# The second layer's first tile also computes its four hidden blocks with narrower weights (126, 112, 96 columns) and with 256 tokens

## The chip, the core and the metric

The kernel runs on one core of a Trainium2 chip. The metric is the device time in microseconds (us), the median of three runs. On this core TensorE does the products and writes them to PSUM, VectorE (DVE), ScalarE (ACT) and GpSimd (POOL) do the elementwise work, and SyncE (SP) starts the transfers.

## The reference, cut to what matters

Three layers follow each other: a gated linear attention, a gated MLP, and a mixture of four experts in which every token goes through every expert. The change lies in the last of them:

```python
def _moe2_ref(x, domain_probs, w1, w2):          # x 3072 x 384, w1 4 x 384 x 1024, w2 4 x 1024 x 384
    p = domain_probs / (domain_probs.sum(-1, keepdims=True) + 1e-09)
    out = np.zeros((N, D), dtype=np.float32)
    for e in range(E):
        h = np.maximum(x @ w1[e], 0.0)
        out += p[:, e:e + 1] * (h @ w2[e])
    return out
```

## The kernel before, in words

The attention and the MLP (which the kernel's names call layer 1) run interleaved first, in eight tiles of 384 tokens; the mixture of experts (layer 2) follows. Each value that enters a large product is split into a high part, which the product's operand type fp32r keeps, and a low part, the remainder. So `x @ w` is three products: high by high, high by low and low by high (`SPLITS`, line 66).

Layer 2 makes eight passes, one for each half of the hidden width of each of four experts (`expert`, line 658). A pass goes over six tiles of 512 tokens. For each tile TensorE computes four hidden blocks (`first`, line 622: three slices of the model width by three splits, that is nine products with weights of 128 columns against 512 tokens), and between them four result blocks of the tile before (`second`, line 632: twelve products, 384 wide). Each block has its own PSUM bank: `hidden_banks` is (5, 6, 0, 1).

Behind each hidden block, ACT takes the relu as the high part (line 820) and DVE makes the low part (line 993). DVE adds the results to `acc` (line 985). The tokens of a tile are split by ACT (`split_x`, line 781) and by POOL (line 1094); those of the second tile by ACT and by DVE (line 1004).

The first tile of layer 2 is special, and the change lies there. Its blocks 0 and 1 are computed before the last output group of layer 1 (line 593, nine products), by the argument `ahead` of line 675; blocks 2 and 3 come after that group, at the start of `expert(0, alone=True)`. No result block stands between these four. Then TensorE waits for the last copy of layer 1 (`x2_ready`), which is ACT's line 760, and goes on with the second tile: its tokens must be split (`xsh_ready`, `xsl_ready`), and its block 0 waits in `first` (line 624) until DVE has made the first low part of the tile before (`rl_ready`).

Each engine runs its own instructions in order. A product in the trace is a pair: a weight load (LDWEIGHTS, engine "PEld") and the product itself (MATMUL, engine "PE").

Of the kernel before, what the change touches and what calls it, by code (L numbers as in the profile page):

```python
# [33 lines left out]
P = 128  # L34
B, H, S, D = 4, 8, 768, 48
DM = H * D
KD = DM // P
# [25 lines left out]
TILES2 = N // T2  # L63
PASSES = E * (F2 // FH)

SPLITS = ((0, 0), (0, 1), (1, 0))

# [139 lines left out]
def nth(e, c, j, per, extra):  # L209

    return e * (2 * TILES2 * per) + j * (2 * per) + (c * per + extra)


def wait_count(eng, sem, n):

    if not isinstance(n, int) or n > 0:
        eng.wait_ge(sem, n)
# [10 lines left out]
def attention_moe_program(nc, qk, alpha, v, rows, w_gate, w_val, w_out, probs, w1, w2, masks, eye, out):  # L228
    with ExitStack() as ctx:
# [4 lines left out]
        start = (nc.sbuf_base + 31) // 32 * 32  # L234
# [4 lines left out]
        def sb(name, shape, dt=F32):  # L239
            t = nc.alloc_sbuf_tensor_at(name, shape, dt, offset=top[0])  # L240
            top[0] += (int(np.prod(shape[1:])) * 4 + 31) // 32 * 32
            assert top[0] <= start + slab_bytes, (name, top[0] - start - slab_bytes)
            return t
# [37 lines left out]
        W1 = [[sb(f"W1_0{c}", [P, KD, FH], F32R) for c in "hl"]]  # L281
        W2 = [[sb(f"W2_0{c}", [P, FCH, DM], F32R) for c in "hl"]]
        XS = [[sb(f"XS_0{c}", [P, KD, T2], F32R) for c in "hl"]]
# [25 lines left out]
        PS = ctx.enter_context(nc.psum_tensor("PS", [P, 8, 512], F32))  # L309
        gate_bank, value_bank, out_bank0, att_bank0 = 0, 1, 2, 5  # L310
        hidden_banks = (5, 6, 0, 1)
# [200 lines left out]
        def _(pe):  # L512
# [57 lines left out]
            def group(i, tc, kind, f):  # L570
# [3 lines left out]
                if kind in ("gate", "value"):  # L574
# [6 lines left out]
                    for n in range(KD):  # L581
                        for w, x in SPLITS:
                            mm = pe.matmul(PS[:, bank, 0:T1], W[w][:, n, f * P:(f + 1) * P], xT[p][x][:, n, :],  # L583
                                           start=(n == 0 and (w, x) == SPLITS[0]), stop=(n == KD - 1 and (w, x) == SPLITS[-1]))
                    mm.then_inc(done, 1)
# [5 lines left out]
                for n in range(KD):  # L591
                    for w, x in SPLITS:
                        mm = pe.matmul(PS[:, out_bank0 + n, 0:T1], WO[w][:, f, n * P:(n + 1) * P], hs[f % 2][x][:],  # L593
                                       start=(f == 0 and (w, x) == SPLITS[0]), stop=(f == FC1 - 1 and (w, x) == SPLITS[-1]))
                mm.then_inc(out_done, 1)
# [26 lines left out]
            def first(e, c, j, f):  # L622

                wait_count(pe, rl_ready, nth(e, c, j, FCH, f + 1 - FCH))
                for n in range(KD):
                    for w, x in SPLITS:
                        mm = pe.matmul(PS[:, hidden_banks[f], :], W1[c // TILES2][w][:, n, f * P:(f + 1) * P],  # L627
                                       XS[c % 2][x][:, n, :],
                                       start=(n == 0 and (w, x) == SPLITS[0]), stop=(n == KD - 1 and (w, x) == SPLITS[-1]))
                mm.then_inc(first_done, 1)  # L630
# [11 lines left out]
            def tile2(e, c, j=0, alone=False, pieces=range(FCH)):  # L642

                if c % TILES2 == 0 and 0 in pieces:
                    pe.wait_ge(w1_ready, e * 2 + (c // TILES2 + 1))
                pe.wait_ge(xsh_ready, nth(e, c, j, 1, 1))
                pe.wait_ge(xsl_ready, nth(e, c, j, 1, 1))
                for f in pieces:
                    first(e, c, j, f)
                    if alone:  # L650
                        continue
                    if f == 0:
                        if (c - 1) % TILES2 == 0:
                            pe.wait_ge(w2_ready, e * 2 + ((c - 1) // TILES2 + 1))
                        pe.wait_ge(rl_ready, nth(e, c, j, FCH, 0))
                    second(e, c - 1, j, f)
# [561 lines left out]
```

## Time and profile before

| | us |
|---|---|
| Time, median of 3 runs (lowest to highest) | 1490.44 (1489.59 to 1491.31) |
| Time of the profiled execution | 1493.83 |
| Its span, from first to last instruction | 1492.0 |
| TensorE products busy in it | 1438.6 (96%) |
| Span from 686 us on (layer 2) | 806.0 |
| TensorE products busy in layer 2 | 803.04 |

A program on one core is timed here by its whole device time; the profile's span is the part between its first and last instruction. Records of products overlap: a product's record lasts 0.33 or 0.39 us while the next one starts 0.17 or 0.23 us after it. So the pace is read from starts, not from durations.

### The profile page before, as it was taken

The page shows a single profiled execution, that of the slowest core. Times are in us where ns is not written, and L with a number is a line of the kernel's source. Part 1 is how long each engine was busy: PE and PEld are TensorE (multiplying, and loading weights), DVE is VectorE, ACT ScalarE, POOL GpSimd, SP SyncE. Part 2 cuts the span into 40 slices and gives each one's busy share as a digit, 9 for nine tenths or more (in the row PEclk, how much of TensorE's full clock was granted, in tenths as well). Part 3 has the DMA queues.
Part 4 walks back from the last instruction along what each step waited for, and adds up shares of the span by engine and source line. Part 5 has one row for each costly group of instructions (what it writes and reads, how often), then busy time and mean ns, then how long its engine had stood idle before and what let it go on. Part 6 is the DMA issues. An engine that isn't in the chain of part 4 may idle for free.

```text
span 1492.0 us, 25792 instructions
## 1 busy us (share of the span) xinstructions
PE 1438.6 (96%) x10296; PEld 1327.3 (89%) x10296; DVE 620.4 (42%) x908; ACT 501.0 (34%) x975; POOL 597.8 (40%) x570
## 2 busy tenths in 40 slices
PE   3799999999999999999999999999999999999999
PEld 3688999898999898999999999999999999999998
DVE  8766654646455555312333333333333333333332
ACT  5554444545445445322222222222222222222220
POOL 7666454544444535254423413323234133242120
PEclk9999999999999999999999999999999999999999
DMA  6512122112121212100001001010010010100011
GB/s 229 188 51 102 51 84 70 68 67 70 66 88 52 93 60 83 43 22 22 0 1 43 0 1 43 0 43 1 1 42 0 0 42 0 42 0 0 19 44 63
DMA packets 31115, 70.70 MB, mean 47 GB/s; under 512 B 5168, under 2 KB 14128, under 8 KB 31024
## 3 DMA queue, kind: packets, MB, share of 16 engines
q1 hardware_dynamic: 31024, 69.43, 13.6%
q8 instruction: 64, 1.05, 0.3%
q14 instruction: 27, 0.22, 0.0%
HBM read 64.70 MB, written 4.72 MB: 47 GB/s over the span
## 4 chain that ended last, share of the span: by engine, by line
PE 89%; DVE 5%; issue 2%; POOL 2%; ACT 1%; DMA 1%; SPq 0%; DVEq 0%; ACTq 0%; POOLq 0%
PE PS L637 27%; PE PS L627 27%; PE PS L583 19%; PE PS L593 9%; PE PS L531 3%; PE PS L554 1%; DVE KQ L861 1%; PE PS L550 1%; ACT QX L738 1%; PE PS L534 1%; DVE near L866 1%; DMA V<-in_v 1%; DVE KQ L846 1%; DVE TOT L855 1%; DMA KQ<-in_qk 0%
## 5 line engine op out<-in xcount | busy, mean ns | idle before, releaser
L1094 POOL TENSOR_TENSOR XS_0l<-x2T,XS_0h 128x1536 fp32r<-128x1536 f32 x24 | 84.4, 3516 | 261.5 <-ACT XS_0h L781 261.5
L985 DVE SCALAR_TENSOR_TENSOR acc<-PS,prob,acc 128x384 f32<-128x384 f32 x192 | 118.7, 618 | 160.5 <-PE PS L637 160.5
L1094 POOL TENSOR_TENSOR XS_1l<-x2T,XS_1h 128x1536 fp32r<-128x1536 f32 x23 | 80.7, 3509 | 250.6 <-ACT XS_1h L781 250.6
L738 ACT ACTIVATE QX<-KQ 48x256 f32<-48x256 f32 x288 | 120.8, 419 | 139.5 <-DVE KQ L846 102.9
L820 ACT ACTIVATE H_1h<-PS 128x512 fp32r<-128x512 f32 x96 | 57.4, 598 | 309.9 <-PE PS L627 309.9
L820 ACT ACTIVATE H_0h<-PS 128x512 fp32r<-128x512 f32 x96 | 57.2, 598 | 297.3 <-PE PS L627 297.2
L846 DVE TENSOR_TENSOR KQ<-KQ,TOT 112x512 f32<-112x512 f32 (+1 forms) x144 | 126.9, 891 | 66.2 <-PE PS L531 37.7
L993 DVE SCALAR_TENSOR_TENSOR H_1l<-PS,H_1h 128x512 fp32r<-128x512 f32 x96 | 66.4, 691 | 195.8 <-ACT H_1h L820 195.8
L993 DVE SCALAR_TENSOR_TENSOR H_0l<-PS,H_0h 128x512 fp32r<-128x512 f32 x96 | 66.1, 691 | 187.4 <-ACT H_0h L820 187.4
L531 PE MATMUL PS<-QX,KQ 112*64 112x64 f32 x1920 | 86.7, 237 | 41.2 <-ACT QX L738 36.2
L531 PEld LDWEIGHTS PS<-QX,KQ 112*64 112x64 f32 x1920 | 73.2, 148 | 56.8 <-issue 27.9
L929 DVE TENSOR_TENSOR hid<-PS,hid 128x384 f32<-128x384 f32 x96 | 53.5, 557 | 155.9 <-PE PS L583 152.8
L1063 POOL TENSOR_TENSOR hs0l<-hid,hs0h 128x384 fp32r<-128x384 f32 x48 | 52.7, 1098 | 125.0 <-ACT hs0h L755 125.0
L1063 POOL TENSOR_TENSOR hs1l<-hid,hs1h 128x384 fp32r<-128x384 f32 x48 | 49.2, 1025 | 129.9 <-ACT hs1h L755 129.9
L751 ACT ACTIVATE hid<-PS 128x384 f32<-128x384 f32 x96 | 47.1, 491 | 80.2 <-PE PS L583 79.2
L1024 POOL TENSOR_TENSOR TOT<-TOT 112x128 f32<-112x128 f32 (+1 forms) x144 | 56.9, 395 | 26.4 <-DVE TOT L855 17.0
L894 DVE COPY_PREDICATED AT<-mask,PS 128x512 f32<-128x512 int32 x72 | 65.9, 915 | 0.5
L637 PE MATMUL PS<-W_1l,H_0h 128*128 128x384 f32 x192 | 64.8, 337 | 0.0
L637 PE MATMUL PS<-W_0l,H_1h 128*128 128x384 f32 x192 | 64.7, 337 | 0.0
L637 PE MATMUL PS<-W_1h,H_0h 128*128 128x384 f32 x192 | 64.7, 337 | 0.0
L637 PE MATMUL PS<-W_0h,H_1h 128*128 128x384 f32 x192 | 64.6, 337 | 0.0
L637 PE MATMUL PS<-W_0h,H_0h 128*128 128x384 f32 x192 | 64.6, 337 | 0.0
(152 smaller groups left out, 4137.1 us busy)
## 6 DMA issues: line engine op xcount, KB each, us to landing
row<-in_rows SPq DMA_DIRECT2D x24, 768.0 KB, 4.3
KQ<-in_qk SPq DMA_DIRECT2D x24, 448.0 KB, 4.1
V<-in_v SPq DMA_DIRECT2D x24, 384.0 KB, 4.8
rawA<-in_w SPq DMA_DIRECT2D x8, 768.0 KB, 4.8
rawB<-in_w SPq DMA_DIRECT2D x8, 768.0 KB, 6.4
A<-in_alpha SPq DMA_DIRECT2D x24, 224.0 KB, 2.7
out_y<-acc SPq DMA_DIRECT2D x5, 768.0 KB, 3.5
raw<-in_w_gate SPq DMA_DIRECT2D x3, 768.0 KB, 8.4
```

Source lines behind the costliest of these rows:

```text
L531: mm = pe.matmul(dst[mine, :, right], KQ[p][0:R, 1, a, mine], cols[:, :, right], start=True, stop=True)
L583: mm = pe.matmul(PS[:, bank, 0:T1], W[w][:, n, f * P:(f + 1) * P], xT[p][x][:, n, :], start=(n == 0 and (w, x) == SPLITS[0]), stop=(n == K ...
L593: mm = pe.matmul(PS[:, out_bank0 + n, 0:T1], WO[w][:, f, n * P:(n + 1) * P], hs[f % 2][x][:], start=(f == 0 and (w, x) == SPLITS[0]), stop ...
L627: mm = pe.matmul(PS[:, hidden_banks[f], :], W1[c // TILES2][w][:, n, f * P:(f + 1) * P], XS[c % 2][x][:, n, :], start=(n == 0 and (w, x) = ...
L637: mm = pe.matmul(PS[:, result_banks[u], 0:DM], H2[c % 2][x][:, f, u * P:(u + 1) * P], W2[c // TILES2 % 2][w][:, f, :], start=(f == 0 and ( ...
L738: done = nc.scalar.activation(QX[p][rows, :, g, :].rearrange("d a (n t) -> d a n t", t=2 << level), right, ACT.Copy)
L820: nc.scalar.activation(H2[c % 2][0][:, f, :], PS[:, hidden_banks[f], :], ACT.Relu).then_inc(rh_ready, 1)
L846: dve.tensor_tensor(x, x, y, ALU.mult).then_inc(kq_ready[p], 1)
L985: dve.scalar_tensor_tensor(out=acc[:, n, :], in0=PS[:, result_banks[u], 0:DM], scalar=weight, in1=acc[:, n, :], op0=ALU.mult, op1=ALU.add) ...
L993: dve.scalar_tensor_tensor(out=low, in0=PS[:, hidden_banks[f], :], scalar=0.0, in1=high.bitcast(F32), op0=ALU.max, op1=ALU.subtract).then_ ...
L1063: nc.gpsimd.tensor_tensor(hs[f % 2][1][:], hid[f % 2][:], hs[f % 2][0][:].bitcast(F32), ALU.subtract).then_inc(hl_ready, 1)
L1094: nc.gpsimd.tensor_tensor(XS[c % 2][1][:], x2T[:, :, at:at + T2], XS[c % 2][0][:].bitcast(F32), ALU.subtract).then_inc(xsl_ready, 1)
```

## The change

In `first`, after the wait on `rl_ready` and ahead of the usual nine products, the first tile of the first pass (expert 0, tile 0) also issues nine products for each of its four blocks: block 0 with the first 126 columns of its weight slices, block 1 with 112, block 2 with 96, all against 512 tokens, and block 3 with all 128 columns against the first 256 tokens. They write the same bank as the usual products; the usual group begins with `start=True`, and so overwrites what they left. No wait and no signal is added.

```diff
+FIRST_COLUMNS = ((126, 512), (112, 512), (96, 512), (128, 256))
 ...
             def first(e, c, j, f):
 
                 wait_count(pe, rl_ready, nth(e, c, j, FCH, f + 1 - FCH))
+                for cols, wide in FIRST_COLUMNS[f:f + 1] if isinstance(e, int) and e + c == 0 else ():
+                    for n in range(KD):
+                        for w, x in SPLITS:
+                            pe.matmul(PS[0:cols, hidden_banks[f], 0:wide], W1[c // TILES2][w][:, n, f * P:f * P + cols],
+                                      XS[c % 2][x][:, n, 0:wide], start=(n == 0 and (w, x) == SPLITS[0]),
+                                      stop=(n == KD - 1 and (w, x) == SPLITS[-1]))
                 for n in range(KD):
                     for w, x in SPLITS:
                         mm = pe.matmul(PS[:, hidden_banks[f], :], W1[c // TILES2][w][:, n, f * P:(f + 1) * P],
```

## Rows read from the trace of the kernel before

**Rows 1.** The page: TensorE's busy time, and its granted clock in 40 slices.
```profile
PE 1438.6 (96%) x10296; PEld 1327.3 (89%) x10296; DVE 620.4 (42%) x908; ACT 501.0 (34%) x975; POOL 597.8 (40%) x570
...
PEclk9999999999999999999999999999999999999999
```
**Rows 2.** The page: the chain that ended last, shares of the span by line.
```profile
PE PS L637 27%; PE PS L627 27%; PE PS L583 19%; PE PS L593 9%; PE PS L531 3%; PE PS L554 1%; DVE KQ L861 1%; PE PS L550 1%; ACT QX L738 1%; PE PS L534 1%; DVE near L866 1%; DMA V<-in_v 1%; DVE KQ L846 1%; DVE TOT L855 1%; DMA KQ<-in_qk 0%
```
**Rows 3.** Windows: layer 2 (busy us and count of each engine, clock, DMA).
```profile
686.00:1492.00 806.00, 803.04 (x4042) 728.27 (x4040) 252.79 (x385) 180.33 (x240) 250.11 (x151) 1.00 0.05 19
```
**Rows 4.** TensorE's waits after 686 us: total, times, longest.
```profile
PEld PS L627 <- issue: 0.4, 1, 0.4
```
**Rows 5.** Chain in order of time, 686 to 702 us: start, us, what.
```profile
686.05 4.09 PE PS L627 x18
690.14 1.56 PE PS L593 x9
691.70 4.09 PE PS L627 x18
695.79 0.05 issue
695.84 2.32 PE PS L627 x9
...
700.25 2.08 PE PS L627 x9
```
**Rows 6.** TensorE's timeline from 178.4 us: transposes in plain fp32 between products.
```profile
178.46 0.34 PE L593 MATMUL PS<-hs0h,WOl 128*128 128x384 f32 x1
178.64 0.49 PE L567 MATMUL PS<-ident,ynat 128*128 128x128 f32 x3
```
**Rows 7.** Groups by form: the transposes of line 567, busy us, mean ns.
```profile
L567 PE MATMUL PS<-ident,ynat 128*128 128x128 f32 x72 | 12.2, 278 | 2.0 <-DVE ynat L902 2.0
```
**Rows 8.** From 178.4 us too, weight loads.
```profile
178.46 0.43 PEld L567 LDWEIGHTS PS<-ident,ynat 128*128 128x128 f32 x3
```
**Rows 9.** The same kind of place with line 539, from 171.2 us.
```profile
171.24 0.34 PE L593 MATMUL PS<-hs1h,WOl 128*128 128x384 f32 x1
171.43 0.55 PE L539 MATMUL PS<-ident,KQ 112*128 112x112 f32 x4
```
**Rows 10.** From 300.7 us: a product, then one with 64 weight columns.
```profile
300.76 0.34 PE L593 MATMUL PS<-hs0h,WOl 128*128 128x384 f32 x1
301.03 0.30 PE L550 MATMUL PS<-ST,KQ 112*64 112x96 f32 x2
```
**Rows 11.** The weight loads there.
```profile
301.03 0.20 PEld L550 LDWEIGHTS PS<-ST,KQ 112*64 112x64 f32 x4 [0.25 <-DMA V<-in_v]
```
**Rows 12.** The weight load of the second tile's first product.
```profile
695.81 0.19 PEld L627 LDWEIGHTS PS<-XS_1h,W_0h 128*128 128x128 f32 x1 [0.44 <-issue]
```
**Rows 13.** TensorE's timeline around the second tile's first product: start, us.
```profile
695.40 0.39 PE L627 MATMUL PS<-XS_0h,W_0l 128*128 128x512 f32 x1
695.84 0.47 PE L627 MATMUL PS<-XS_1h,W_0h 128*128 128x512 f32 x1
696.15 0.40 PE L627 MATMUL PS<-XS_1l,W_0h 128*128 128x512 f32 x1
```
**Rows 14.** ACT's timeline, then DVE's, 690 to 697 us.
```profile
691.74 1.49 ACT L781 ACTIVATE XS_1h<-x2T 128x1536 fp32r<-128x1536 f32 x1 [5.97 <-PE PS L593]
693.13 1.12 ACT L760 ACTIVATE x2T<-PS 128x1152 f32<-128x1152 f32 x1
694.14 2.28 ACT L820 ACTIVATE H_0h<-PS 128x512 fp32r<-128x512 f32 x4
...
693.33 1.76 DVE L1004 TENSOR_TENSOR XS_1l<-x2T,XS_1h 128x1536 fp32r<-128x1536 f32 x1 [8.18 <-ACT XS_1h L781]
695.01 2.48 DVE L993 SCALAR_TENSOR_TENSOR H_0l<-PS,H_0h 128x512 fp32r<-128x512 f32 x4
```
**Rows 15.** The page: group of DVE's line 993: busy us, mean ns of one.
```profile
L993 DVE SCALAR_TENSOR_TENSOR H_0l<-PS,H_0h 128x512 fp32r<-128x512 f32 x96 | 66.1, 691 | 187.4 <-ACT H_0h L820 187.4
```

## The prediction

> **What bounds the kernel now.** I read the page first. TensorE's products are busy for 96% of the span at the full clock, and no other engine comes to half of it [rows 1]. The chain that ended last is made of TensorE's lines, with 27% each for the two lines of layer 2 [rows 2]. The windows then show layer 2 by itself: 803 of its 806 us are busy with products, at a granted clock of 1.00, which is the 2.4 GHz level [rows 3]. The list of waits has a single entry for TensorE in that whole stretch, 0.4 us at a weight load of line 627 [rows 4]. So from 686 us on TensorE is the bound with no slack under it: a product put in there moves the end by its own pace, and only that one wait can give something back. The chain in order of time shows the place of the change [rows 5]. Blocks 0 and 1 of the first tile take 4.09 us (18 products), then come layer 1's last nine products (1.56), blocks 2 and 3 (4.09), a short stop, and the second tile.
>
> **What is added.** The condition (a Python integer `e`, with e + c = 0) holds for the first tile of the first pass alone, once for each of four blocks: 4 x 9 = 36 products with their weight loads, 27 against 512 tokens and nine against 256. All are on TensorE, in a stretch where its starts follow each other without a gap. They sit on the path with their full price.
>
> Pace of the usual kinds: 4.09 / 18 = 0.2272 us for 512 tokens, 1.56 / 9 = 0.1733 for 384 [rows 5]. 128 tokens more cost 0.0539 us, so 384 of them are 0.1617, and 0.0116 is left that does not depend on the tokens: some 0.012 us for each pair of load and product.
>
> *Nine products against 256 tokens.* The columns are the usual 128. By the same line, 0.1733 - 0.0539 = 0.1194 us each, 1.07 us for nine. Could pairs follow each other that fast? The nearest row is a run of three transposes with 128 columns against 128: 0.49 us long [rows 6], one of them 0.278 [rows 7], so (0.49 - 0.28) / 2 = 0.105 us apart. That is just below 0.119, so I take 1.07. From below, the tokens alone are 9 x 0.108 = 0.97; from above, if a pair needed as long as one at 384 tokens, 9 x 0.1733 = 1.56.
>
> *27 products against 512 tokens with 126, 112 and 96 columns.* If the number of columns did not matter they would cost 27 x 0.2272 = 6.13 us: narrower weights leave columns of the array idle and do not shorten the stream of tokens. What may change is the load. No row of this kernel shows a load of fp32r weights with fewer than 128 columns, so I bound it from both sides.
> - From below: the load costs nothing, and the fixed 0.012 goes too: 27 x 0.2156 = 5.82 us.
> - The nearest row with another kind of load: the three plain fp32 transposes after a 384-token product. Their first load starts with that product, at 178.46 [rows 8], and the transpose starts 0.18 us after it [rows 6], where the usual distance is 0.173; with line 539 it is 0.19 [rows 9]. So a full-width load of the other type is hidden beside the running product but for some 0.01 us more than usual. 27 x 0.01 = 0.27.
> - From above: a load that cannot start until the stream before it has ended. The trace has one with 64 columns, where load and product start together in the records, 0.27 us after the product before [rows 10, 11], that is 0.10 us above the usual 0.173. The one exposed load of layer 2 agrees: from its start at 695.81 [rows 12] to the second product at 696.15 [rows 13] is 0.34 us, a product's 0.227 and 0.11 before it. 27 x 0.10 = 2.7 us.
>
> I take the middle one, because its load fills the whole array as these nearly do, whereas that of rows 10 changes over to half of it (and part of its wait is put down to a DMA). So the narrow products cost 6.13 + 0.27 = 6.40 us.
>
> Here the Trainium skill speaks against the change being that cheap. Its page "TensorE: Matmul & The Clock Gate", section "Weight-path perf modes — Fast Weight Load (FWL) and DoubleRow", says in my words that the fast load is used only when there are exactly 128 weight columns of a type other than fp32, and in theory loads them four times as fast. By that rule blocks 0 to 2 leave the fast load and block 3 keeps it, with the same page's "LDWEIGHTS" section giving columns / 1.2 in ns (105, 93 and 80 ns). Fully exposed, that would make the narrow products about 27 x 0.09 = 2.5 us dearer; fully hidden, nothing. No row here shows the fast load being left for this type.
>
> **What goes.** The one stop of layer 2. The first product of the second tile starts 0.44 us after the one before it and the next 0.31 after that [rows 13], against 0.227 each: 0.21 + 0.08 = 0.29 us lost (the chain has the same: 0.05 of issue, and 2.32 where a block otherwise takes 2.08 [rows 5]). The profile names no releaser; the code and the rows do. Block 0 of the second tile waits for the first low part of the first tile. After layer 1's last group ends (691.7), ACT splits the second tile until 693.2, DVE makes its low part from 693.33 to 695.09, and only then the first low part, from 695.01 on, 0.69 us long [rows 14, 15]: it is done at 695.70, and the load starts 0.11 later. This chain is 4.0 us long from the end of layer 1's last group, and TensorE has 4.09 us of products to lay beside it, of which the load ahead takes the margin. The added products of blocks 2 and 3 stand in the same place and make that 4.09 + 9 x 0.237 + 1.07 = 7.3 us. The wait goes: -0.29 us. The added products of blocks 0 and 1 come before layer 1's last group and shift both sides alike.
>
> What is late next? The low part of block 3, which the first result block waits for. ACT's 0.57 (2.28 / 4 [rows 14]) and DVE's 0.69 us [rows 15] after the end of block 3's last product, whose record of 0.39 us reaches 0.16 into the second tile, give 1.4 us; the load that wants it comes 8 products, 1.8 us, in. It holds, with 0.4 us to spare; without this cover it would cost a few tenths. ACT, DVE and POOL follow TensorE's signals afterwards as before and are idle most of the time. No transfer is touched: nothing of SP's and POOL's queues is moved past anything.
>
> **The sum.** 6.40 + 1.07 - 0.29 = +7.18 us. The profiled execution took 1493.83 us (span 1492.0 and 1.8 around it) and would take 1501.0. It lies 3.4 us above the median of the runs shown, and since nothing here scales with that difference, I carry the sum over: 1490.44 + 7.18 = 1497.6 us.
>
> **The rivals.**
> - *The load becomes a serial term, one step for each column.* The fixed 0.012 us may be a load that is never hidden and is fast for full-width weights only. If narrow weights went in one column at a time, at the pace at which tokens stream (0.0539 us for 128), 126, 112 and 96 columns would take 0.053, 0.047 and 0.040 us in place of the 0.012: 9 x (0.041 + 0.035 + 0.028) = 0.94 us above 6.13. Sum 6.13 + 0.94 + 1.07 - 0.29 = +7.85, time 1498.3. For it: the fixed part is there at both widths [rows 5]. Against it: in rows 8 a full-width load of another type, though nothing says that it is a fast one, was nearly hidden. By the fast-load rule of the page named above, four times 0.012 is 0.047 for a full-width load, which is what this rival takes for 112 columns; the rows neither bear out nor exclude it.
> - *Every narrow load is exposed as in rows 10.* 6.13 + 2.7 + 1.07 - 0.29 = +9.6, time 1500.1. For it: those are the only rows with fewer than 128 columns that follow an fp32r product. Against it: their switch to half the array, and a queue of TensorE that issues the next load at the start of the running product everywhere else.
> - *The narrow products leave the fast product too*, and stream at the pace of the plain fp32 rows: 0.105 us for 128 tokens [rows 6, 7], twice 0.054. Then 27 products cost 27 x 0.44 = 11.9, and with 1.07 and -0.29 the sum is +12.7, time 1503.1. Only the transposes speak for it, and these are bound by their loads as well as by their tokens.
> - *Not slower.* Layer 2 runs a little behind its own best pace: a hidden block takes 2.04 us in the quiet stretch (4.09 / 2) but 2.08 later [rows 5]. Over some 48 tiles with four such blocks these 0.04 us are 7.7 us. If the slow pace came from how the other engines' accesses fall against TensorE's, and the shift of 7 us moved them apart for good, it would give back up to 7.7 and end at 7.18 - 7.7 = -0.5, time 1489.9. It would have to give back over 4.2 us to leave "slower". Against it: the other engines wait for TensorE's signals, so they are shifted with it.
> - *The products are not there*, or write in parallel with others: they would need to be dropped or run beside the usual ones. They use the same array and bank, so I give this nothing of its own.
>
> **Chances.** My forecast 0.60 (1496.9 with the load free, to 1497.9), the serial load 0.19, the exposed load 0.10, the slow stream 0.07, not slower 0.04. Range: from 1496.4 (load free, and half a microsecond for the spread of the runs) to 1500.2, which takes in the exposed load. What a measurement of this kernel can tell from no change is about 0.2%, 3.0 us. Only the last rival comes under that: faster 0.01, same 0.03, slower 0.96.
>
> **What would show it right or wrong.** The rows of the new line should be 36 products and 36 loads between 685.9 and some 703 us. The distance of starts should be 0.23 to 0.24 us in the three narrow groups, about 2.13 us for nine, with no fall from 126 to 112 to 96, and 0.12 us in the fourth. Distances that fall with the columns (0.269, 0.262, 0.256) show the serial load, 0.32 or more the exposed one, 0.43 the slow stream. The wait of rows 4 should be gone and the distance at the second tile's start be 0.23. The rest of layer 2 should be as long as before. Any difference over 1 us outside the first 20 us of layer 2 would make the whole sum wrong.

## The result, and the profile after

The changed kernel takes 1498.54 us (median of three, 1498.43 to 1501.93) against 1490.44 (1489.59 to 1491.31): a ratio of 1.0062, 95% interval 1.0038 to 1.0085. The forecast was 1497.6 us, in a range of 1496.4 to 1500.2. A second comparison gave 1.0050 (1.0032 to 1.0067); it stands below with the experiments.

The medians differ by 8.1 us, and the two profiled executions by less: 1498.54 against 1493.83 us, spans 1496.8 against 1492.0. The trace says why. It has to be read in two parts, from the first product of the kernel to layer 2's first product, and from there to the last product of the kernel:

| us, from starts of products in the trace | before | after |
|---|---|---|
| first product to layer 2's first | 677.98 | 675.63 |
| layer 2's first product to the last of the kernel | 802.865 | 809.925 |

The trace of the kernel after has 36 products more (10332 against 10296). The second row is the change, +7.06 us. It is the same to the last digit in a second profile of the changed kernel (809.925). The first row is work that the change doesn't touch, and it scatters: over the thirteen profiles of this study it lies between 673.9 and 681.7 us.

The chain of the kernel after in order of time (start, us, what) answers to [rows 5]. Line 629 is the added product, 634 the usual hidden block (627 before), 594 layer 1's last output group (593 before), 644 the result block.

```profile
683.71 2.10 PE PS L629 x9
685.81 2.06 PE PS L634 x9
687.86 2.06 PE PS L629 x9
689.93 2.04 PE PS L634 x9
691.97 1.57 PE PS L594 x9
693.53 2.08 PE PS L629 x9
695.61 2.04 PE PS L634 x9
697.65 1.07 PE PS L629 x9
698.73 4.15 PE PS L634 x18
```

The four added groups stand there with 2.10 us (126 columns), 2.06 (112), 2.08 (96) and 1.07 (256 tokens), 7.31 in all. The piece of 4.15 us is block 3 of the first tile and block 0 of the second: there is no "issue" piece between them, and the list of waits has no entry for TensorE any more in layer 2 where [rows 4] had one. The starts around the second tile's first product (answering to [rows 13]) show the same:

```profile
700.40 0.39 PE L634 MATMUL PS<-XS_0h,W_0l 128*128 128x512 f32 x1
700.63 0.40 PE L634 MATMUL PS<-XS_1h,W_0h 128*128 128x512 f32 x1
700.87 0.40 PE L634 MATMUL PS<-XS_1l,W_0h 128*128 128x512 f32 x1
```

0.23 us from start to start in both places, where it was 0.44 and 0.31. ACT, then DVE, in the same stretch (answering to [rows 14]):

```profile
693.57 1.49 ACT L788 ACTIVATE XS_1h<-x2T 128x1536 fp32r<-128x1536 f32 x1 [10.14 <-PE PS L594]
694.97 1.11 ACT L767 ACTIVATE x2T<-PS 128x1152 f32<-128x1152 f32 x1
695.98 1.07 ACT L827 ACTIVATE H_0h<-PS 128x512 fp32r<-128x512 f32 x2
...
695.16 1.76 DVE L1011 TENSOR_TENSOR XS_1l<-x2T,XS_1h 128x1536 fp32r<-128x1536 f32 x1 [12.35 <-ACT XS_1h L788]
696.84 1.28 DVE L1000 SCALAR_TENSOR_TENSOR H_0l<-PS,H_0h 128x512 fp32r<-128x512 f32 x2
...
701.46 0.69 DVE L1000 SCALAR_TENSOR_TENSOR H_0l<-PS,H_0h 128x512 fp32r<-128x512 f32 x1 [2.45 <-ACT H_0h L827]
```

The split's low part is done at 696.9 and the first low part at 697.5, over 3 us ahead of the product at 700.63. The last low part ends at 702.15, and the weight load of the first result block, which needs it, starts at 702.48: what is late next stayed covered, with 0.3 us to spare. (The chain gives that block's start as 702.88, because it counts from the end of the record before; its first product starts at 702.71.)

The bill of layer 2, from starts in the two traces: added groups +7.31; the stop gone -0.28 (0.435 to 0.228 and 2.155 to 2.083 for the nine products behind it); the usual groups beside the added ones 8.21 instead of 8.18, +0.03. Sum, from the unrounded starts, +7.06.

### The profile page after: what moved, and what is told of

Read it like the earlier page. It is cut to its first block, busy times and chain, and to the rows that moved or that the text cites. A ratio compares the mean times of both kernels' runs of the same rounds, so it can differ in the third digit from the quotient of the medians.

```text
span 1496.8 us, 25864 instructions
## 1 busy us (share of the span) xinstructions
PE 1444.6 (97%) x10332; PEld 1332.2 (89%) x10332; DVE 622.8 (42%) x908; ACT 500.9 (33%) x975; POOL 597.0 (40%) x570
## 4 chain that ended last, share of the span: by engine, by line
PE 90%; DVE 5%; ACT 2%; issue 2%; DMA 0%; SPq 0%; DVEq 0%; ACTq 0%
PE PS L644 27%; PE PS L634 27%; PE PS L584 19%; PE PS L594 9%; PE PS L532 3%; PE PS L555 1%; ACT QX L745 1%; PE PS L551 1%; DVE KQ L868 1%; DVE near L873 1%; PE PS L535 1%; DVE KQ L853 1%; DVE TOT L862 1%; PE PS L540 1%; PE PS L629 0%
## 5 line engine op out<-in xcount | busy, mean ns | idle before, releaser
L853 DVE TENSOR_TENSOR KQ<-KQ,TOT 112x512 f32<-112x512 f32 (+1 forms) x144 | 130.2, 915 | 65.7 <-PE PS L532 37.6
```

What stands on the lines that cost most here:

```text
L853: dve.tensor_tensor(x, x, y, ALU.mult).then_inc(kq_ready[p], 1)
```

## The experiments

Eleven runs follow. "Layer 2" is from its first product to the last product of the kernel, from starts in the trace. Where a kernel ran only once, only the trace is used, since the first part of the kernel moves the device time by some us.

### Full width in all four blocks (one run)

```diff
-FIRST_COLUMNS = ((126, 512), (112, 512), (96, 512), (128, 256))
+FIRST_COLUMNS = ((128, 512), (128, 512), (128, 512), (128, 512))
```

> All four added blocks with 128 weight columns against 512 tokens, so that only the width differs from the changed kernel in blocks 0 to 2. Theory (the width of the weights does not matter while 512 tokens stream over them): the added groups of nine take 2.10, 2.06 and 2.08 us as they did with 126, 112 and 96 columns, each within 0.02, and the usual groups stay as they were. Rival (narrow loads pay a little that the neighbours hide, 1 to 4 ns a product): the full-width groups take 2.04 to 2.05 us, the best pace of this kernel, 0.03 to 0.05 less than the narrow ones. Block 3 takes 2.04 to 2.08 instead of 1.07. Layer 2 from its first product to its last: 809.9 + 1.0 = 810.9 us by the theory, 810.8 by the rival; the device time 1 us above the changed kernel's, within the spread of the first part of the kernel.

The chain of this kernel:

```profile
684.27 2.05 PE PS L629 x9
686.32 2.04 PE PS L634 x9
688.36 2.04 PE PS L629 x9
690.40 2.04 PE PS L634 x9
692.44 1.56 PE PS L594 x9
694.00 2.05 PE PS L629 x9
```

Layer 2 took 810.746 us. The rival was right by a small amount: full width takes 2.05, 2.04 and 2.05 us where 126, 112 and 96 columns took 2.10, 2.06 and 2.08. So the narrow groups took 6.23 - 6.15 = 0.09 us more together (unrounded), 0.003 for each of 27 products, and saved nothing. The sweep at the end puts in doubt that this is a price of the width.

### Narrow weights against 256 tokens (one run)

```diff
+FIRST_COLUMNS = (((126, 256), (128, 256)), ((112, 256),), ((96, 256), (64, 256)), ((128, 256),))
-                for cols, wide in FIRST_COLUMNS[f:f + 1] if ...
+                for cols, wide in FIRST_COLUMNS[f] if ...
```

> Added products against 256 tokens: block 0 with 126 and then 128 columns, block 1 with 112, block 2 with 96 and then 64, block 3 with 128. Theory (a load runs beside the product before it and only a fixed 0.012 us is left): 0.119 to 0.12 us from start to start for every width. Rival (a load of fewer than 128 columns is slower, and was hidden only because 512 tokens take 0.213 us): at 256 tokens, 0.107 us of streaming, the narrow widths come out longer than 0.12, up to 0.15 to 0.18 for 126, 112 and 96 columns, shrinking with the columns, while 128 columns stay at 0.12. A second rival for 64 columns (half of the array, as in the rows of line 550): the first product after a change of width class costs 0.10 us more.

The nine products of each kind took 1.058 us (126 columns), 1.080 (128), 1.057 (112), 1.045 (96), 1.030 (64) and 1.072 (128 again). From start to start that is 0.114 to 0.120 us. No narrow load is exposed at 256 tokens either; narrow is faster here by up to 0.006 us a product. Both rivals fell, and the theory's 0.119 to 0.12 us for every width missed by that much.

### Narrow weights against 128 tokens and less (one run)

```diff
+FIRST_COLUMNS = (((128, 128), (126, 128)), ((112, 128), (128, 192)), ((96, 128), (64, 128)), ((126, 192), (128, 64)))
```

The loop is changed as in the run before; this holds for every list of lists below.

> Added products against few tokens. Block 0: 128 columns x 128 tokens, 126 x 128. Block 1: 112 x 128, 128 x 192. Block 2: 96 x 128, 64 x 128. Block 3: 126 x 192, 128 x 64. Theory (fixed 0.012 us and the streaming alone, without a floor): 0.066 us from start to start at 128 tokens, 0.093 at 192, 0.039 at 64, whatever the columns. Rival A (a load and its product cannot follow the next pair faster than a floor of 0.105 to 0.11 us, as the transposes and the one exposed load of the kernel before): all of these at 0.105 to 0.11. Rival B (the floor exists and is higher for fewer than 128 columns): 128 columns 0.07 to 0.11, 126, 112 and 96 columns longer than 128 at the same tokens, in the order of their columns. Rival C (fp32r falls to a slower product under 256 tokens): 0.2 us or more for 128 and 192 tokens at every width.

This is the run that shows the load. The timeline of TensorE (start, record's length, what), all against 128 tokens, for 126, 112, 96 and 64 columns:

```profile
688.63 0.28 PE L629 MATMUL PS<-XS_0h,W_0h 128*126 128x128 f32 x1
...
689.18 0.27 PE L629 MATMUL PS<-XS_0h,W_0l 128*126 128x128 f32 x1
...
691.90 0.26 PE L629 MATMUL PS<-XS_0h,W_0l 128*112 128x128 f32 x1
...
692.40 0.26 PE L629 MATMUL PS<-XS_0l,W_0h 128*112 128x128 f32 x1
...
697.43 0.25 PE L629 MATMUL PS<-XS_0h,W_0l 128*96 128x128 f32 x1
...
697.85 0.25 PE L629 MATMUL PS<-XS_0l,W_0h 128*96 128x128 f32 x1
...
698.14 0.22 PE L629 MATMUL PS<-XS_0h,W_0l 128*64 128x128 f32 x1
...
698.50 0.22 PE L629 MATMUL PS<-XS_0h,W_0l 128*64 128x128 f32 x1
```

The pairs are five products apart (six for 64 columns): 0.55 / 5 = 0.110 us a product with 126 columns, 0.50 / 5 = 0.100 with 112, 0.42 / 5 = 0.084 with 96, 0.36 / 6 = 0.060 with 64. With 128 columns the median distance was 0.112 against 128 tokens, 0.111 against 192 and 0.112 against 64, so between these counts the tokens do not matter. The theory (0.066 us at 128 tokens, whatever the columns) fell. Rival A was right that a floor exists, and it was not one number: it goes with the columns, by about (0.112 - 0.084) / 32 = 0.0009 us each between 128 and 96.

That this floor is the load of the weights can be read from the start of the first group, with 128 columns against 128 tokens:

```profile
687.68 0.22 PE L629 MATMUL PS<-XS_0h,W_0h 128*128 128x128 f32 x1
687.68 0.19 PEld L629 LDWEIGHTS PS<-XS_0l,W_0h 128*128 128x128 f32 x1
687.74 0.28 PE L629 MATMUL PS<-XS_0l,W_0h 128*128 128x128 f32 x1
687.79 0.19 PEld L629 LDWEIGHTS PS<-XS_0h,W_0l 128*128 128x128 f32 x1
687.85 0.27 PE L629 MATMUL PS<-XS_0h,W_0l 128*128 128x128 f32 x1
```

The second product follows the first by only 0.058 us. The next load starts 0.11 us after the one before it, and from there on each product keeps that distance. So the products could go at 0.058, and the loads hold them back. With 64 columns the distance, 0.060, is about that of the tokens: each load there starts with the running product again, as against 512 tokens, so this row does not show how long a 64-column load takes. A load of 128 columns is no faster for its full width than one of 126 (0.112 and 0.110), so rival B had the order the wrong way round, and rival C fell.

Against 512 tokens, 0.216 us of streaming by the prediction's slope (4 x 0.0539), such a load has room beside the product before it. This is why the change's narrow weights neither save nor cost much. The rule weighed in the prediction (the Trainium skill, "TensorE: Matmul & The Clock Gate", "Weight-path perf modes — Fast Weight Load (FWL) and DoubleRow", which gives its four times as a theory for fp8) would make the 128-column load faster than that with 126 if it held for fp32r; the runs do not show it for this type, and the measurement decides. The same page's "LDWEIGHTS" section gives columns / 1.2 in ns: 106.7 for 128 and 80 for 96, and the trace agrees with its 112 and 84 to some 4 to 5 ns.

### The added products of blocks 0 and 1 alone (one run)

```diff
+FIRST_COLUMNS = (((126, 512),), ((112, 512),), (), ())
```

> The added products of blocks 0 and 1 alone (126 and 112 columns); none for blocks 2 and 3. Theory (the stop at the second tile's first product is a chain of 4.0 us that starts with the end of layer 1's last output group, and the added products of blocks 2 and 3 cover it): with none there, the stop is back, 0.44 us and 0.31 between the starts there, 0.29 us lost, and layer 2 takes 802.87 + 2.10 + 2.06 = 807.0 us from its first product to its last. Rival (the stop was a hiccup of issuing, or came from anything before layer 1's last group): no stop, 806.7 us.

```profile
694.86 1.56 PE PS L594 x9
696.42 4.09 PE PS L634 x18
700.51 0.04 issue
700.55 2.31 PE PS L634 x9
702.87 2.08 PE PS L644 x12
```

The stop is back, with 0.432 and 0.313 us between the starts, although TensorE had 4.16 us more to do ahead of layer 1's last group. So it belongs to what begins with that group's end, and the added products of blocks 2 and 3 are what covers it. Layer 2 took 806.41 us, 0.6 less than the 807.0 expected. That missing part lies behind the second tile's start: from there to the end it takes 792.29 us here, and 792.84 in the four other kernels above. See the last section.

### Four times the dose at 512 tokens (one run)

```diff
+FIRST_COLUMNS = (((126, 512),) * 4, ((128, 512),) * 4, ((96, 512),) * 4, ((64, 512), (64, 512), (32, 512), (32, 512)))
```

> Four times nine added products against 512 tokens in each block: block 0 with 126 columns, block 1 with 128, block 2 with 96, block 3 with 64 and 64 and 32 and 32. Theory (the load of any width is hidden under 512 tokens): every group of nine takes 2.04 to 2.10 us, so 36 with 126 columns take 8.2 to 8.4 and 36 with 96 columns the same; 16 groups add 33 to 33.5 us to layer 2, whose second-tile stop is gone: 802.9 + 33.2 - 0.3 = 835.8 us. Rival A (the fixed part is a quarter of a step per column, as the runs at 256 tokens hint: 128 columns 0.120, 64 columns 0.1135): 96 columns 0.2233 (2.01 us for nine), 64 columns 0.220 (1.98), 32 columns 0.2167 (1.95), 126 columns 2.04. Rival B (126 columns cost 0.233 us a product, 0.006 above full width, as in its one group so far, for as long as they go on): block 0 takes 36 x 0.233 = 8.39 us against 8.16 for block 1.

```profile
683.06 8.40 PE PS L629 x36
...
693.52 8.16 PE PS L629 x36
...
705.29 8.29 PE PS L629 x36
...
715.63 8.31 PE PS L629 x36
```

36 products took 8.40 us with 126 columns, 8.16 with 128, 8.29 with 96, 8.31 with 64 and 32. Layer 2 took 835.79 us, as expected (835.8). Rival B was right for 126 columns: 0.233 us each for as long as they go on. Rival A fell: fewer columns do not save time here.

### The dose at 256 tokens (one run)

```diff
+FIRST_COLUMNS = (((128, 256),) * 3 + ((64, 256),) * 3, ((32, 256),) * 3, ((96, 256),) * 3, ((112, 256),) * 3)
```

> Added products against 256 tokens, 27 in a row of each width: 128 and then 64 columns in block 0, 32 in block 1, 96 in block 2, 112 in block 3. Theory (a fixed part of 0.012 us whatever the columns): 0.119 us each, 3.22 us for 27 of any width. Rival (the fixed part goes with the columns, a quarter of a step for each): 128 columns 0.1200 (3.24 us for 27), 112 columns 0.1183 (3.20), 96 columns 0.1167 (3.15), 64 columns 0.1133 (3.06), 32 columns 0.110 (2.97). A third possibility (no order at all, 0.112 to 0.121 as in the mixed groups before): differences that don't follow the columns.

For nine products: 1.080 us with 128 columns, 1.060 with 112, 1.044 with 96, 1.020 with 64, as the rival has it to 0.01, but 1.060 with 32, where it wants 0.99. So the rival does not hold for all of them, and at 512 tokens it had the wrong sign. The theory's one time for all widths missed too. What sets these last 0.006 us a product stays open.

### The changed kernel again (seven runs)

> The changed kernel again, timed in five rounds against the kernel before on one chip. Theory (7.1 us come from layer 2, in every run, and anything else is the scatter of the first part of the kernel, whose half-clock windows and waits differ from run to run): +7.1 us between the medians give or take the scatter, a ratio of 1.0048 with an interval that may reach from 1.002 to 1.008; layer 2 809.9 us from its first product to its last in the profile. Rival (the change itself also makes the first part slower, by some 1 us, as 8.1 between the medians of three would have it): 1.0054 or more, and a first part longer than that of the kernel before.

1499.12 us (1497.32 to 1504.8, seven runs) against 1493.46 (1489.92 to 1496.94, eighteen runs); ratio 1.0050, 1.0032 to 1.0067. Layer 2 took 809.925 us in the profile, and the first part 678.03 us, as long as before's 677.98 in its own profile. The theory holds: 7.06 of 1490.44 us is 1.0047, inside both intervals, and the second comparison comes close to it. The rival's 1.0054 lies inside them too; what speaks against it is the first part, which isn't longer in the profile.

### Relu and low part of block 0 first, nothing added (twelve runs)

```diff
                 act.wait_ge(out_done, TILES1 * FC1)
+                act.wait_ge(first_done, 1)
+                nc.scalar.activation(H2[0][0][:, 0, :], PS[:, hidden_banks[0], :], ACT.Relu).then_inc(rh_ready, 1)
                 act.wait_ge(x2_ready, 2)
                 split_x(0, 1)
 ...
```

and the same for DVE's low part, ahead of its line 1004; both are left out of the usual loops.

> The kernel before with nothing added, but with the relu (ACT) and the low part (DVE) of the first tile's block 0 put ahead of the second tile's split. Theory (the stop of 0.29 us is the wait for the first low part at the end of a chain of 4.0 us): that low part is ready 1.4 us after layer 1's last group instead of 4.0, the split's low part takes its place at 0.6 + 1.5 + 1.8 = 3.9 us, and the stop shrinks to 0.1 us or none: layer 2 802.6 to 802.8 us from its first product to its last, the time the same as before (0.3 of 1490 us is 0.02%). Rival (the wait is one for the split, which now comes later by 0.6 us): the stop grows to 0.5 us or more, layer 2 803.2.

Ratio 1.0007 (0.9997 to 1.0017). Layer 2 took 802.858 us: the stop stayed (0.431 and 0.312 us), so the theory failed, and so did the rival's longer stop. DVE's timeline and the chain show what took over:

```profile
692.66 0.69 DVE L1005 SCALAR_TENSOR_TENSOR H_0l<-PS,H_0h 128x512 fp32r<-128x512 f32 x1 [7.22 <-ACT H_0h L810]
694.11 1.76 DVE L1009 TENSOR_TENSOR XS_1l<-x2T,XS_1h 128x1536 fp32r<-128x1536 f32 x1 [0.75 <-ACT XS_1h L781]
```
```profile
696.09 0.04 issue
696.13 2.31 PE PS L627 x9
```

The first low part was ready at 693.35, but the split's low part, which the relu in front of it had pushed back, now ended at 695.87. Both kernels can be compared by the time since the first product of block 2 (691.54 in the kernel before, 691.84 here). There the last low part needed ended 4.15 us after it, here the split's ended 4.04 after it, 0.12 us sooner; the load at which TensorE stops starts 4.27 us after it in both. Where the 0.12 us went stands in the trace's records of TensorE's own waiting instructions, of which no view is shown here: the wait for the split's low part comes one instruction ahead of that for the first low part. It goes through 0.04 us after the low part's end, the second waiting instruction follows 0.11 us later, and the load 0.08 after that. In the kernel before, the low part that came last was the second instruction's, which went through 0.04 us after it, with only the 0.08 behind. So moving one producer up pushed the other back to nearly the same time, and the order of the waits took the rest.

### The split in thirds as well (eleven runs)

```diff
-                split_x(0, 1)
+                for k in range(KD):
+                    nc.scalar.activation(XS[1][0][:, k, :], x2T[:, k, T2:2 * T2],
+                                         ACT.Copy).then_inc(xsh_ready if k == KD - 1 else xs_part, 1)
 ...
```

This stands on top of the edit of the run before, and DVE makes its low part in the same three pieces.

> The kernel before with nothing added, the relu and low part of the first tile's block 0 first (as in the run before this), and the second tile's split made in three pieces, one for each slice of the model width, so that DVE makes the low part of a slice while ACT makes the high part of the next. Theory (the stop ends with whichever comes last of the first low part and the split's low part; the one was moved before and the other, 4.04 us after layer 1's last group, took its place): the split's low part is now ready some 3.4 to 3.6 us after that group, before the 3.87 us at which TensorE could issue the load, and the stop is gone: 0.227 us from start to start there, layer 2 802.57 us from its first product to its last. Rival (the stop is TensorE's own cost of taking three waits in a row at that place): 0.43 and 0.31 us stay, 802.86. The time is the same as before in either case: 0.3 of 1490 us is 0.02%.

Ratio 1.0004 (0.9994 to 1.0014).

```profile
691.75 0.69 DVE L1008 SCALAR_TENSOR_TENSOR H_0l<-PS,H_0h 128x512 fp32r<-128x512 f32 x1 [7.22 <-ACT H_0h L811]
692.36 1.89 DVE L1013 TENSOR_TENSOR XS_1l<-x2T,XS_1h 128x512 fp32r<-128x512 f32 x3
695.25 1.89 DVE L998 SCALAR_TENSOR_TENSOR H_0l<-PS,H_0h 128x512 fp32r<-128x512 f32 x3 [1.00 <-ACT H_0h L825]
```
```profile
691.08 6.17 PE PS L628 x27
697.25 0.03 issue
697.28 2.32 PE PS L638 x12
```

The 27 products of blocks 2 and 3 and the second tile's block 0 now run without a stop: with both conditions ready, at 692.4 and 694.25, the wait is gone. That shows that it was these two, and the rival, a cost of TensorE's own, fell. But the stop has moved: the first result block waits for the fourth low part, which DVE ends at 697.14. The new stop loses as much as the old one (0.422 and 0.247 us, where 0.227 and 0.174 are usual: 0.27). Layer 2 took 802.232 us, 0.63 less than before, and 0.59 of that is the pace of the last section.

### Two relus first (eleven runs)

The run before, with block 1's relu and low part put ahead of the split too (two lines for each engine).

> As the run with the split in thirds, and the relu and low part of block 1 are also put ahead of the split, so that less is left for DVE behind it. Theory (in the run before, the first stop went and a second took its place: the first result block waits for the fourth low part, which DVE had ready 6.06 us after layer 1's last group, where TensorE could use it at 5.9): the fourth low part is now ready at 5.5 to 5.7 us and no stop is left, layer 2 802.23 - 0.27 = 801.96 us from its first product to its last. Rival (the last copy of layer 1 on ACT, pushed to 3.7 us, becomes what TensorE waits for at 3.87): a stop of 0.1 to 0.3 us at the second tile's first product, 802.1 to 802.3. The time stays within what can be told from the kernel before: 0.9 of 1490 us is 0.06%.

Ratio 0.9995 (0.9983 to 1.0007). The theory fell: a stop stands at the second tile's first product again, with 0.318 and 0.312 us between the starts, 0.18 lost, and layer 2 took 802.745 us. The size of the stop is the rival's, its cause is not. The view of waits puts it down to the last copy of layer 1:

```profile
PEld PS L628 <- ACT x2T L761: 0.3, 1, 0.3
```

But that entry goes by the load's own wait alone, and the split's low part (DVE) ended later than the copy (ACT):

```profile
697.29 1.13 ACT L761 ACTIVATE x2T<-PS 128x1152 f32<-128x1152 f32 x1
...
696.58 1.89 DVE L1016 TENSOR_TENSOR XS_1l<-x2T,XS_1h 128x512 fp32r<-128x512 f32 x3
```

The copy ends at 698.42, the split's low part at 698.47, and the load starts at 698.70, 0.23 us behind the low part, the same distance as in the run with one relu first (695.87 and 696.10). TensorE's waiting instruction for that low part goes through 0.04 us after its end, with the same 0.11 and 0.08 us behind it. The copy was only 0.05 us from being the last. The two relus and low parts put ahead had pushed both back. None of the three reordered kernels is faster than the one before by more than its measurement can tell.

### Token counts between 320 and 504 (one run)

```diff
+FIRST_COLUMNS = (((126, 504), (128, 504), (126, 448), (128, 448)), ((126, 384), (128, 384), (96, 384), (64, 384)),
+                 ((126, 320), (128, 320), (96, 320), (64, 320)), ((96, 448), (64, 448), (96, 504), (64, 504)))
```

> Added products with 126, 128, 96 and 64 columns against 504, 448, 384 and 320 tokens, nine of each. Theory (streaming plus a fixed 0.0133 us for 128 columns; at 512 tokens the narrower ones showed up to 0.0066 us more, at 256 up to 0.0066 us less): 128 columns 0.2233, 0.200, 0.1733 and 0.1467 us. For the others two readings: (A) the extra at 512 tokens belongs to the width, and is there at every token count above some point: 126 columns 0.230, 0.2065, 0.180, 0.153; (B) it comes from how load and stream fall against each other in steps of 0.0033 us, and changes with the token count without order: some of the counts show 126 columns at the pace of 128 or below it. In neither case is any load exposed: nothing above 0.24 us at 504 tokens.

Nine products took, in us, with 128 / 126 / 96 / 64 columns: 2.062 / 2.048 / 2.069 / 2.057 against 504 tokens, 1.824 / 1.815 / 1.830 / 1.825 against 448, 1.562 / 1.590 / 1.574 / 1.564 against 384, 1.313 / 1.318 / 1.318 / 1.315 against 320. Reading B fits: 126 columns are faster than 128 at 504 and 448 tokens and slower at 320, 384 and 512, so the 0.006 us at 512 are hardly the price of a narrow load. Each number is from a single group of nine, in one order, so an effect of the place in the row isn't excluded. All lie within 2% of full width. The theory's size missed at 504 tokens even for 128 columns: 2.01 us expected, 2.062 measured.

## Why the prediction was right, point by point

*The bound.* Right. Layer 2 paid for each added product in full, and beside the stop nothing else in it moved by more than 0.03 us.

*256 tokens, 1.07 us.* Measured 1.07. The doubt whether pairs can follow at 0.119 us was well placed: a 128-column load takes 0.111 to 0.112 us, as the run with few tokens shows, and that is the 0.11 of the exposed load of [rows 12, 13]. Whether the 0.105 of the transposes, which are of another type, is the same thing was not tried.

*27 narrow products, 6.40 us.* Measured 6.23. The mechanism was right (a load without a special width is hidden beside the product before it), and the term was mis-sized: I charged 0.01 us a product from the transposes, where 0.003 were measured against full width. The picture is simpler than the three cases that I bounded: a full-width load is no faster than a narrow one, and both are hidden from 256 tokens on, but for differences of some ns that stay open.

*The stop, -0.29 us.* Measured -0.28, and the cause named, the wait for the first low part, fits the kernel before: it ended at 695.70 and the split's low part 0.6 us ahead of it. The two runs that took the cover away or took the conditions away agree: without the added products of blocks 2 and 3 the stop is back, and with both conditions early it is gone. What I did not see is that the split stands in the same chain, so that moving the low part alone gains nothing. For the change itself this made no difference, since the added 3.15 us in blocks 2 and 3 cover both.

*What is late next.* Right: no wait came up. The low part of block 3 was ready 0.3 us before the load that needs it, where 0.4 were predicted.

*The sum, +7.18 us.* Measured +7.06 in layer 2. The difference of 8.1 us between the medians of three is this and 1 us of scatter in the first part; the range held it because of the room left for the exposed load, not because I had sized the scatter. That part is luck: in the second comparison the medians differ by 5.7 us, and 1490.44 + 5.7 would have been 1496.1, just under the range. I wrote off the 3.4 us between the profiled execution and the median, and should have read it as that scatter: the kernel before lay between 1489.3 and 1496.9 us over all its runs in this study.

*The rivals.* The serial load is out: it would show 0.269, 0.262 and 0.256 us, and 0.233, 0.229 and 0.231 were measured. The exposed load is out: 32 and 64 columns against 512 tokens took 0.230 to 0.232 us, where it asks for 0.32. So [rows 10] (64 columns of plain fp32) show something else; what it is wasn't tried. The slow stream is out. "Not slower" is out: 7.06 us stayed, though a change of pace like the one it spoke of exists in small (last section).

## What to carry to other kernels

A product added on the engine that is the bound costs its whole distance from start to start, here 0.23 us against 512 tokens. Making its weights narrower saves nothing at 512 tokens and costs next to nothing, as long as the stream is longer than the load, here 0.11 us for 128 columns. With 192 tokens and fewer a 128-column load set the pace, and at 128 tokens fewer columns did help, down to 64. When a stop is removed by moving one producer up, look for the other conditions that end within a few tenths of it, and for the order in which the waiting engine takes them: this stop was ended by the first low part, then by the split's, then (at another place) by the fourth low part, then by the split's again with layer 1's last copy 0.05 us behind it. Check the view of waits against the ends of all producers: it named the copy, which was not the last.

## What the runs showed of the hardware that was not expected

The distance between two equal products is not one number. For 512 tokens with 128 columns it lies between 224 and 236 ns in layer 2 of the kernel before, in patterns that depend on what stands around the products, and some patterns last as long as nothing disturbs them: 36 products at a mean of 233 ns with 126 columns, 230 with 96, and 227 with 128. Such a pattern can tip for a while. From the second result block to the end of the kernel the same instructions take 786.59 us in eleven of the thirteen profiles, to 0.001 us, and 786.00 in two: the kernel with added products in blocks 0 and 1 only, and the split in thirds. The whole difference arises in the first 80 us of that stretch, about the first pass; from there on the starts keep the same distance to 0.001 us. At its beginning the result blocks have 2.08 us instead of 2.09 in the chain, and the hidden blocks 2.06 instead of 2.08. What picks the one or the other was not tried and stays open; it is worth 0.59 us here, twice the stop.
